# A longer warm-up of TensorE ahead of x, in float32r, with its moving data read in eight orders

## The chip, the cores and the metric

The kernel runs on one NeuronCore of a Trainium2 chip. The metric is the device time of one execution in microseconds (us), lower is better. The profile is that of one execution; its span runs from the first to the last instruction.

## The reference

`x` has the shape (2, 3008, 256). It goes through the real part of a two-dimensional Fourier transform and then, as 6,016 tokens of 256 features, through two feed-forward layers:

```python
X = np.fft.fft(np.fft.fft(x, axis=1), axis=2).real           # (2, 3008, 256)
rms = np.sqrt(np.mean(x * x, axis=-1, keepdims=True) + 1e-06) # x is now X as (6016, 256)
xn = x / rms * rms_g
g, val = xn @ w_gate, xn @ w_val                              # 256 x 1536 each
x = (g * (1 / (1 + np.exp(-g))) * val) @ w_out                # 1536 x 256
h = x @ w_in                                                  # 256 x 2048
out = (h * np.cos(h)) @ w_out2                                # 2048 x 256
```

## The kernel before

Each engine has a stream of its own, written out by hand, and semaphores order them. The stages that the prediction speaks of are these.

*Warm-up and loads.* SyncE issues ten loads of `x` (with the first table in front, the tile `front`), then the other tables and w1b, w1a, none of which waits for compute. VectorE clears a tile `zeros` of 128 columns (L928) and a single value of `stat` (L929). TensorE waits for `zeros_ready` and runs `warm_up(15)`: 15 float32 products of zeros by zeros, 128 columns each, into PSUM bank 7 (L465). A float32 product shows in the profile as two records.

*First transform along the sequence* (the first stage). VectorE folds each chunk of x as it lands (L934, L941, L944). TensorE multiplies the folded chunks, 24 pairs of rows in nine groups (L492, and L488/L489 where a chunk is only half folded), each product with 136 moving columns in float32. `warm_up(2)` stands ahead of the second and the third chunk. ScalarE copies each group out of one of six PSUM banks (L694) and turns a row of it (L702); for the last groups VectorE does part of this (L951, L959).

*Features and second transform.* Once all groups are out, TensorE runs, for each of 34 steps, the transform over features (L508) and along the sequence (L524, L526), and sums of squares (L548), all float32. In the same stretch ScalarE, VectorE and GpSimd split the first layer's weights in a high and a low float32r part.

*Main loop.* Six tiles of 502 pairs of tokens. Each product of the two layers is made of three float32r products (L561, L562, L563: high by high, high by low, low by high) of 502 moving columns. This begins at about 55 us and takes the rest of the span.

The SBUF address of `zeros` is that of buffers used later (`plus0`, one of the `pq` buffers). The moving operand of every product in this kernel is contiguous along its columns.

Of the kernel before, what the change touches and what calls it, by code (L numbers as in the profile page):

```python
# [6 lines left out]
F32 = mybir.dt.float32  # L7
F32R = mybir.dt.float32r
# [3 lines left out]
P = 128  # L12
# [12 lines left out]
N = PAIRS // PER_BATCH  # L25
# [52 lines left out]
def build(nc, x, w1a, w1b, small, wo1, win2, wo2, t_feat, t_seq2, t_const, out):  # L78
    ctx = ExitStack()
    with ctx:  # L80
# [5 lines left out]
        def sb(name, shape, at, dt=F32):  # L86
            return nc.alloc_sbuf_tensor_at(name, [P] + shape, dt, offset=base + at)
# [72 lines left out]
        o_pq = o_h + 4 * TA  # L160
        pq = [sb(f"pq{i}", [DIM], o_h + UVB + 1024 * i if i < 3 else o_pq + 2048) for i in range(4)]
        assert UVB + 3 * 1024 <= 4 * TA and 4 * N <= 2048
        zeros = sb("zeros", [P], o_pq)
        plus = [sb("plus0", [N], o_pq), sb("plus1", [N], o_x2 + 1024)]
        assert o_work + 4 * GCOLS <= o_x2 + 1024 and o_x2 + 1024 + 4 * N <= o_hid - UVB
        o_end = o_pq + pad(max(TB, 16 * DIM))
# [12 lines left out]
        ps = ctx.enter_context(nc.psum_tensor("ps", [P, 8, 512], F32))  # L179
# [24 lines left out]
        root_ready, zeros_ready = sem("root_ready"), sem("zeros_ready")  # L204
# [57 lines left out]
        def mean_rows(q):  # L262
            return sum(k.stop - k.start for _, k in PART_ROWS[:q + 1])
# [196 lines left out]
        @block.tensor  # L460
        def _(pe):

            def warm_up(count):
                for _ in range(count):
                    nc.tensor.matmul(ps[:, 7, 0:P], zeros[:, :], zeros[:, :], start=True, stop=True)  # L465

            pe.wait_ge(zeros_ready, 1)
            warm_up(15)
            pe.wait_ge(x_in[0], 16)
            for g, ms in enumerate(GROUPS):  # L470
                for i, m in enumerate(ms):
                    if m in CHUNK_AT:
                        if m:
                            warm_up(2 if CHUNK_AT.index(m) < 3 else 0)
                        pe.wait_ge(folded, CHUNK_AT.index(m) + 1)
                        if CHUNK_AT.index(m) == HALF_FOLDED[0]:
                            pe.wait_ge(seq1_turned, 4)
                    for c in group_order(g):
                        if i == 0 and g >= 3 and c == 0:
                            pe.wait_ge(n1_out, g - 2)  # L480
                        if i == 0 and g >= 3 and c == 1:
                            pe.wait_ge(row_turned, 2 * (g - 2))
                        if m == 0 and c:
                            pe.wait_ge(seq1_turned, 2)
                        acc = ps[:, n1_bank(g, c), i * COLS1:(i + 1) * COLS1]
                        even, odd = (x_sb[:, m * XM + r * P:m * XM + (r + 1) * P] for r in range(2))
                        if half_folded(m):
                            nc.tensor.matmul(acc, even, seq1_thirds[c], start=True, stop=False)  # L488
                            last = nc.tensor.matmul(acc, odd, seq1_thirds[2 * c],  # L489
                                                    start=False, stop=True)  # L490
                        else:
                            last = nc.tensor.matmul(acc, odd if c else even, seq1_thirds[c],  # L492
                                                    start=True, stop=True)
                        if i == len(ms) - 1:
                            last.then_inc(n1_done, 1)
# [429 lines left out]

        @block.vector
        def _(dve):
            nc.vector.memset(zeros[:, :], 0.0).then_inc(zeros_ready, 1)  # L928
            nc.vector.memset(stat[0:1, 0, 0:1], 1.0).then_inc(root_ready, 1)  # L929
            for i in range(XL):  # L930
                dve.wait_ge(x_in[i], 16)
# [394 lines left out]
```

## Time and profile before

| | us |
|---|---|
| median of 2 runs | 979.88 (978.4 to 981.35) |
| span of the profiled execution | 976.5 |
| warm-up, L465, first to last record's end | 1.07 to 7.12 |
| first stage on TensorE | 7.35 to 22.32 |
| features and second transform | 23.22 to 54.85 |
| main loop | 54.85 to the end |

PE is TensorE's matmuls and PEld its weight loads, DVE is VectorE, ACT ScalarE, POOL GpSimd and SP SyncE. L465 is line 465 of the kernel. A matmul record lasts longer than the distance to the next start, since matmuls overlap; the distance between starts is what one costs in a dense stream.

### The profile page before, as it was taken

The numbers are of one execution on the slowest core, as the hardware profiler recorded it, in microseconds if no ns is written. First come the engines' busy times: TensorE is split into PE (matmuls) and PEld (weight loads), VectorE is DVE, ScalarE is ACT, GpSimd is POOL, SyncE is SP. The second block draws the span as 40 slices with busy tenths as digits, with TensorE's granted clock in tenths as the row PEclk, the third lists the DMA queues.
The fourth block names the chain that finished last, engine by engine and source line by source line (L and its number), as shares of the span: only waits on it lengthen the run. The fifth ranks groups of instructions, "written<-read, shape, count | busy, mean of one in ns | idle before, by whom it ended". The sixth has DMA issues, their size and how long they took to land.

```text
span 976.5 us, 13031 instructions
## 1 busy us (share of the span) xinstructions
PE 970.6 (99%) x4530; PEld 808.5 (83%) x4530; DVE 741.0 (76%) x1029; ACT 638.4 (65%) x806; POOL 351.3 (36%) x291
## 2 busy tenths in 40 slices
PE   9999999999999999999999999999999999999998
PEld 8988888888888888888888888888888888888886
DVE  7988887678876768876768877767887667887665
ACT  5687687764378765368775358775348776447777
POOL 0477782047720027740007750006661004770000
PEclk9999999999999999999999999999999999999999
DMA  9888010000010001010001010001010000000001
GB/s 354 234 195 247 1 42 12 1 9 35 1 42 1 1 1 42 1 42 0 0 0 42 0 32 11 0 0 42 0 32 0 0 0 21 21 0 0 0 0 42
DMA packets 13794, 36.80 MB, mean 38 GB/s; under 512 B 2586, under 2 KB 6522, under 8 KB 13370
## 3 DMA queue, kind: packets, MB, share of 16 engines
q1 hardware_dynamic: 11690, 31.63, 9.3%
q0 software_dynamic: 2064, 4.72, 2.7%
q8 instruction: 15, 0.25, 0.1%
q14 instruction: 25, 0.20, 0.1%
HBM read 22.35 MB, written 9.26 MB: 32 GB/s over the span
## 4 chain that ended last, share of the span: by engine, by line
PE 97%; DMA 1%; SPq 0%; DVE 0%; ACT 0%; issue 0%
PE ps L561 31%; PE ps L562 31%; PE ps L563 31%; PE ps L508 2%; DMA front<-x 1%; PE ps L526 1%; PE ps L524 1%; SPq L332 0%; PE ps L548 0%; PE ps L492 0%; ACT g_sb L694 0%; DVE front L934 0%; ACT y_sb L923 0%; DVE front L944 0%; DVE front L941 0%
## 5 line engine op out<-in xcount | busy, mean ns | idle before, releaser
L561 PE MATMUL ps<-h_hi,wo_hi 128*128 128x502 f32 x672 | 261.5, 389 | 0.0
L563 PE MATMUL ps<-h_hi,wo_lo 128*128 128x502 f32 x672 | 261.4, 389 | 0.0
L562 PE MATMUL ps<-h_lo,wo_hi 128*128 128x502 f32 x672 | 261.2, 389 | 0.0
L1144 POOL TENSOR_TENSOR h_lo<-work,h_hi 128x502 fp32r<-128x502 f32 x92 | 102.0, 1117 | 371.6 <-ACT h_hi L822 369.8
L807 ACT ACTIVATE h_hi<-work 128x502 fp32r<-128x502 f32 x132 | 82.3, 626 | 176.7 <-POOL work L1233 176.7
L1131 DVE SCALAR_TENSOR_TENSOR work<-work,ps 128x1004 f32<-128x1004 f32 (+1 forms) x109 | 117.2, 1075 | 94.7 <-ACT work L912 94.3
L1117 DVE SCALAR_TENSOR_TENSOR work<-work,ps 128x1004 f32<-128x1004 f32 (+1 forms) x109 | 116.5, 1074 | 48.4 <-ACT work L898 48.4
L561 PE MATMUL ps<-x_hi,win_hi 128*128 128x502 f32 x384 | 149.9, 390 | 0.0
L562 PE MATMUL ps<-x_lo,win_hi 128*128 128x502 f32 x384 | 149.3, 389 | 0.0
L563 PE MATMUL ps<-x_hi,win_lo 128*128 128x502 f32 x384 | 149.2, 389 | 0.0
L561 PEld LDWEIGHTS ps<-h_hi,wo_hi 128*128 128x128 f32 x672 | 126.2, 188 | 26.9 <-DVE h_lo L1038 0.6
L562 PEld LDWEIGHTS ps<-h_lo,wo_hi 128*128 128x128 f32 x672 | 126.3, 188 | 26.0
L563 PEld LDWEIGHTS ps<-h_hi,wo_lo 128*128 128x128 f32 x672 | 126.3, 188 | 26.0
L1045 DVE SCALAR_TENSOR_TENSOR plus<-u,w,ps 128x502 f32<-128x502 f32 x144 | 105.9, 735 | 51.3 <-PE ps L563 50.7
L898 ACT ACTIVATE work<-ps 128x1004 f32<-128x1004 f32 (+1 forms) x109 | 98.3, 907 | 60.2 <-PE ps L563 59.4
L907 ACT ACTIVATE work<-work 128x1004 f32<-128x1004 f32 (+1 forms) x109 | 102.7, 943 | 31.3 <-DVE work L1117 30.4
L1233 POOL TENSOR_TENSOR work<-work,uv_t 128x502 f32<-128x502 f32 x72 | 99.7, 1411 | 45.0 <-DVE uv_t L1054 45.0
L1038 DVE TENSOR_TENSOR h_lo<-work,h_hi 128x502 fp32r<-128x502 f32 x172 | 114.3, 703 | 1.7 <-ACT h_hi L822 0.4
L561 PE MATMUL ps<-uv_hi,w_hi 128*128 128x502 f32 x288 | 112.6, 391 | 0.0
L562 PE MATMUL ps<-uv_lo,w_hi 128*128 128x502 f32 x288 | 112.0, 389 | 0.0
L563 PE MATMUL ps<-uv_hi,w_lo 128*128 128x502 f32 x288 | 111.9, 389 | 0.0
L822 ACT ACTIVATE h_hi<-work 128x1004 fp32r<-128x1004 f32 (+1 forms) x109 | 101.7, 938 | 14.9 <-PE ps L563 8.7
(96 smaller groups left out, 1269.2 us busy)
## 6 DMA issues: line engine op xcount, KB each, us to landing
out<-y_sb SPq DMA_DIRECT2D x10, 502.0 KB, 3.1
front<-x SPq DMA_DIRECT2D x4, 768.0 KB, 8.8
uv_t<-uv_dram SPq DMA_DIRECT2D x6, 502.0 KB, 3.6
front<-x SPq DMA_DIRECT2D x4, 512.0 KB, 8.9
w_lo<-w_f POOLq DMA_DIRECT2D x4, 512.0 KB, 7.5
wo_raw<-wo SPq DMA_DIRECT2D x1, 2048.0 KB, 10.9
win_raw<-win SPq DMA_DIRECT2D x1, 2048.0 KB, 8.0
raw_b<-w1b SPq DMA_DIRECT2D x3, 512.0 KB, 12.4
```

The lines of the kernel that those rows point to most:

```text
L561: nc.tensor.matmul(acc, w_hi, v_hi, start=start, stop=False)
L562: nc.tensor.matmul(acc, w_hi, v_lo, start=False, stop=False)
L563: return nc.tensor.matmul(acc, w_lo, v_hi, start=False, stop=stop)
L822: nc.scalar.activation(h_hi[j % 2][:, gs, 0:N], work[j % 4][:, gs, :], ACT.Copy).then_inc(hi_done, gs.stop - gs.start)
L898: nc.scalar.activation(work[j % 4][:, gs, :], ps[:, bank_pair(j) + gs.start:bank_pair(j) + gs.stop, 0:N], ACT.Copy, bias=MAGIC).then_inc(r ...
L907: nc.scalar.activation(work[j % 4][:, gs, :], work[j % 4][:, gs, :], ACT.Sin, scale=TURN / 2).then_inc(sin_done, gs.stop - gs.start)
L1038: nc.vector.tensor_tensor(h_lo[j % 2][:, g, 0:N], work[j % 4][:, g, :], h_hi[j % 2][:, g, 0:N].bitcast(F32), ALU.subtract).then_inc(hid_sp ...
L1045: nc.vector.scalar_tensor_tensor(out=plus[m][:, :], in0=u128[:, :], scalar=w128[:, m * C1 + i:m * C1 + i + 1], in1=ps[:, bank_pair(m), 0:N ...
L1117: nc.vector.scalar_tensor_tensor(out=buf, in0=buf, scalar=MAGIC, in1=pair, op0=ALU.subtract, op1=ALU.subtract).then_inc(frac_done, gs.stop ...
L1131: nc.vector.scalar_tensor_tensor(out=buf, in0=buf, scalar=1.0, in1=pair, op0=ALU.subtract, op1=ALU.mult).then_inc(cos_done, gs.stop - gs.s ...
L1144: nc.gpsimd.tensor_tensor(dst, src, hi.bitcast(F32), ALU.subtract).then_inc(s, 1)
L1233: nc.gpsimd.tensor_tensor(work[i % 3][:, g, :], work[i % 3][:, g, :], value[i % 2][:, g, :], ALU.mult).then_inc(h_done[g], 1)
```

## The change

`zeros` becomes a float32r tile of 1,536 columns, and the memset clears all of it. The 15 float32 products of 128 columns become 54 float32r products: 14 of 512 contiguous columns, 5 of 502, 5 of 512, and then five each of 512 columns with a step of two values, in turns of 2, of 4 and of 16 values from two stretches 512 values (2 KB) apart, with a step of three values, and with the same 8 values read 64 times. The two `warm_up(2)` inside the first stage keep 128 columns and become float32r.

```diff
-        zeros = sb("zeros", [P], o_pq)
+        zeros = sb("zeros", [1536], o_pq, F32R)
...
-            def warm_up(count):
+            def warm_up(count, moving=zeros[:, 0:P], width=P):
                 for _ in range(count):
-                    nc.tensor.matmul(ps[:, 7, 0:P], zeros[:, :], zeros[:, :], start=True, stop=True)
+                    nc.tensor.matmul(ps[:, 7, 0:width], zeros[:, 0:P], moving, start=True, stop=True)
+
+            def in_turns(run):
+                return zeros[:, 0:1024].rearrange("p (r k i) -> p k r i", r=2, i=run)[:, 0:256 // run]
 
             pe.wait_ge(zeros_ready, 1)
-            warm_up(15)
+            warm_up(14, zeros[:, 0:512], 512)
+            warm_up(5, zeros[:, 0:N], N)
+            warm_up(5, zeros[:, 0:512], 512)
+            warm_up(5, zeros[:, 0:1024:2], 512)
+            warm_up(5, in_turns(2), 512)
+            warm_up(5, in_turns(4), 512)
+            warm_up(5, in_turns(16), 512)
+            warm_up(5, zeros[:, 0:1536:3], 512)
+            warm_up(5, zeros[:, 0:8].rearrange("p (o i) -> p o i", o=1).broadcast_to([P, 64, 8]), 512)
             pe.wait_ge(x_in[0], 16)
...
-            nc.vector.memset(zeros[:, :], 0.0).then_inc(zeros_ready, 1)
+            nc.vector.memset(zeros[:, :].bitcast(F32), 0.0).then_inc(zeros_ready, 1)
```

## Rows read from the trace of the kernel before

**Rows 1.** The page: span and busy time of each engine.
```profile
span 976.5 us, 13031 instructions
PE 970.6 (99%) x4530; PEld 808.5 (83%) x4530; DVE 741.0 (76%) x1029; ACT 638.4 (65%) x806; POOL 351.3 (36%) x291
```

**Rows 2.** Chain of waits, 0 to 21 us: start, us, what.
```profile
0.75 0.40 SPq L332
...
4.91 14.17 DMA front<-x
...
19.10 0.70 DVE front L934
...
19.82 0.43 DVE front L941
...
20.28 0.44 DVE front L944
...
20.76 0.38 PE ps L492
```

**Rows 3.** Groups by form, 0 to 30 us: | busy us, mean ns | idle before.
```profile
L994 DVE TENSOR_SCALAR raw_b<-raw_b,gvec 128x512 f32<-128x512 f32 x2 | 1.0, 476 | 0.0
...
L928 DVE MEMSET zeros<- 128x128 f32 x1 | 0.2, 165 | 0.8 <-PEq L1318 0.8
...
L929 DVE MEMSET stat<- 1x1 f32 x1 | 0.1, 59 | 0.0
```

**Rows 4.** Timeline of VectorE and TensorE, 0 to 23.9 us: start, us, what [idle before].
```profile
0.85 0.17 DVE L928 MEMSET zeros<- 128x128 f32 x1 [0.85 <-PEq L1318]
...
5.06 0.96 DVE L934 TENSOR_TENSOR front<-front 128x768 f32<-128x768 f32 x1 [4.05 <-DMA front<-x]
...
1.07 6.05 PE L465 MATMUL ps<-zeros 128*128 128x128 f32 x30 [1.07 <-DVE zeros L928]
7.35 1.63 PE L492 MATMUL ps<-front 128*128 128x136 f32 x12 [0.23 <-DVE front L944]
...
14.71 1.09 PE L492 MATMUL ps<-front 128*128 128x136 f32 x8
15.64 0.40 PE L488 MATMUL ps<-front 128*128 128x136 f32 x2
...
20.76 1.72 PE L492 MATMUL ps<-front 128*128 128x136 f32 x12 [0.33 <-DVE front L944]
...
23.22 0.87 PE L508 MATMUL ps<-feat,g_sb 128*96 128x129 f32 x6 [0.74 <-ACT g_sb L694]
```

**Rows 5.** Warm-up records in three windows: duration ns min/median/max, first and last start.
```profile
L465 PE MATMUL ps<-zeros x18: 421/421/581, 1.1 to 4.9; 128*128 128x128 f32 x18
...
L465 PE MATMUL ps<-zeros x23: 414/421/581, 1.1 to 5.9; 128*128 128x128 f32 x23
...
L465 PE MATMUL ps<-zeros x8: 275/275/414, 5.9 to 6.8; 128*128 128x128 f32 x8
```

**Rows 6.** Timeline of ScalarE and VectorE at the first stage's end.
```profile
18.85 0.92 ACT L694 ACTIVATE g_sb<-ps 128x408 f32<-128x408 f32 x2
19.80 0.56 ACT L702 ACTIVATE g_sb<-ps 1x204 f32<-1x204 f32 x2
20.26 0.90 ACT L694 ACTIVATE g_sb<-ps 128x408 f32<-128x408 f32 x2
21.20 0.55 ACT L702 ACTIVATE g_sb<-ps 1x204 f32<-1x204 f32 x2
21.99 0.81 ACT L694 ACTIVATE g_sb<-ps 128x272 f32<-128x272 f32 x3 [0.24 <-PE ps L492]
...
21.40 0.29 DVE L944 SCALAR_TENSOR_TENSOR front<-front 128x128 f32<-128x128 f32 x1
```

**Rows 7.** Windows by stage: busy us (instructions) of each engine, clock, DMA.
```profile
7.34:22.32 14.98, 14.64 (x120) 14.19 (x120) 13.53 (x25) 10.61 (x30) 0.00 (x0) 1.00 1.03 393
...
23.20:54.85 31.65, 31.34 (x304) 29.77 (x305) 27.25 (x56) 20.43 (x39) 17.46 (x18) 1.00 0.87 243
54.85:100.00 45.15, 45.11 (x228) 36.37 (x229) 39.42 (x61) 35.73 (x50) 35.55 (x31) 1.00 0.76 205
100.00:976.50 876.50, 873.33 (x3849) 722.24 (x3848) 657.54 (x879) 568.97 (x681) 298.09 (x240) 1.00 0.04 13
```

**Rows 8.** Waits of TensorE: us in total, times, longest.
```profile
PE ps L465 <- DVE zeros L928: 1.1, 1, 1.1
PE ps L508 <- ACT g_sb L694: 0.7, 1, 0.7
PE ps L492 <- DVE front L944: 0.6, 2, 0.3
PE ps L548 <- issue: 0.3, 1, 0.3
```

**Rows 9.** Chain of waits at the end of the span: start, us, what.
```profile
970.84 0.23 PE ps L562
971.07 0.22 PE ps L563
971.29 0.23 PE ps L561
...
973.10 0.24 PE ps L563
```

## The prediction

> **What bounds the kernel now.** I read the page first, then the chain of waits in order of time, then the timeline of TensorE over the first stage, and last the table of stages. The page gives TensorE 99% of the span [rows 1], but that is an average, and the change sits in the first microseconds, so the question is what ends last there. The chain answers it [rows 2]. Up to 19.1 us it holds no matmul: it is the issue of the ten loads of x, then 14.17 us of transfer, then the last large fold on VectorE (19.10 to 20.72), and only then the matmuls at 20.76. The x transfer sets when the first stage can end. TensorE fits itself around it: the 15 old warm-ups run from 1.07 to about 7.1 while x is on its way, and the first stage follows from 7.35 to 22.32 [rows 4]. After 23.22 the chain is TensorE almost without a break: in the stage 23.20 to 54.85 it is busy for 31.34 of 31.65 us, and for 873.33 of 876.50 us from 100 on [rows 7], while its waits behind the first stage are 0.7 and 0.3 us [rows 8]. So what delays TensorE at 23 us delays the end by nearly the same, and what delays it before that counts only beyond the slack that the first stage has under the x transfer.
>
> **Part 1: the memset.** The tile grows from 128 to 1,536 values a partition. One column took 59 ns and 128 columns took 165 ns, so 0.83 ns a column [rows 3]; 1,536 columns give 0.059 + 1,535 x 0.00083 = 1.34 us. Bounds: 1.30 (the slope alone, nothing fixed, is 1.28) to 1.43 (the 512-column tensor_scalar, 0.93 ns a column [rows 3]). It starts at 0.85, ends at 2.19, and the first product follows 0.05 us behind its end as now (1.02 to 1.07 [rows 4]): 2.24. Behind the memset on VectorE are the 1x1 memset, which releases one ScalarE operation, and the first fold at 5.06, which waits for x [rows 3, 4]. Both are covered until 5.06; without that cover the price would be 1.2 us on each. The larger tile lies over buffers that are written only after products further down TensorE's own queue, so I see no new wait, and SyncE's and GpSimd's queues get nothing and are passed by nothing.
>
> **Part 2: the price of one new product.** It is float32r, 512 columns (five have 502). The main loop issues just such products: 502 columns, starts 0.226 us apart (ten gaps from 970.84 to 973.10 [rows 9]), so 0.450 ns a column and 0.230 us for 512. The old float32 product shows as two records; those of 136 columns start 0.116 us apart (8 in 0.93 us [rows 4]), so 0.232 us a product and 1.71 ns a column. A new product at the full clock costs about what an old one did, and there are 54 in place of 15.
>
> **The clock.** The page gives a granted clock of full speed in every slice, but the records of the warm-up say otherwise: durations of 421 ns for the first 18, 275 ns later, the change between 5.9 and 6.3 us [rows 5]. Up to there 23 records start within 4.85 us; less the longer first one (581 ns for 421) that is 22 gaps of 0.213 us, and behind it they are 0.11: the lower of the two levels (1.2 GHz), then the upper (2.4 GHz). TensorE had run without a gap for about 5.1 us when it rose. The new warm-ups are as dense and also zeros, so I let the clock rise 5.1 us after their start, at 7.35. At the lower level a product of 512 columns costs what the old float32 product of 128 cost there, 2 x 0.213 = 0.43 us (by the ratio of levels from the 0.230: 0.44).
>
> **Part 3: the length of the warm-up.** 5.1 / 0.43 = 12 products at the lower level, up to 7.4 us. The other 42 take 42 x 0.23 = 9.7 us. End at 17.1 us, against 7.1 before. This price takes the moving data's order as free. No matmul of this trace reads its moving data with a step or with jumps, so for the 30 products of the six other orders (step 2, turns of 2, 4 and 16, step 3, the same 8 values again and again) the bounds are: below, nothing extra, as in the contiguous row; above, the float32 rate, 3.8 times, 0.64 us more each, 19.3 us in all. I take nothing, because the values delivered per column are the same four bytes as in the nearest row, and keep both ends.
> The Trainium skill, page "SBUF — State Buffer", section "Specifications (TRN2)", speaks against taking nothing for all: lines of 16 bytes, and at least two hits in each for full bandwidth. By that rule step 2 (two float32 in each line) and the turns would be free and step 3 (1.3 in each) would pay; it gives no price, and no run here shows it yet.
>
> **Part 4: the first stage, late.** It starts at 17.1 + 0.1. It has 112 records (24 pairs of rows by two products, eight more for the four half-folded ones, two records each) at 0.116 = 13.0 us. By 21.7 us the last fold is done [rows 6], well ahead of its use, so the stalls that the stage has now (14.97 us less 13.0 less 8 warm-up records of 0.11 = 1.1 us) go: the stage is no longer bound by x but by TensorE. The four warm-ups inside it (2 + 2) are now float32r of 128 columns: between 0.058 us (by columns) and 0.22 (the float32 price); I take 0.11, 0.44 in all. End: 17.2 + 13.0 + 0.44 = 30.6, against 22.32: **8.3 us late**.
>
> **Part 5: what follows.** ScalarE takes 1.41 us to copy out and turn a group of three (18.85 to 20.26; 1.48 by the sum of its operations [rows 6]) and TensorE 1.39 to fill one. Today the stall at 20.4 us lets it catch up; without it its last copy ends about 0.5 us later behind the last product: +0.5. Against that, loads not gated by compute (the tables, w1a, w1b) land as early as before while their users come 8 us later, and the few gaps of TensorE between 23 and 100 us (0.31 + 0.04 us without a record at all, and some single longer steps) can shrink: -0.5. Both are small and cancel. All else is passed on, since TensorE is the chain. Its clock stays at the upper level: it works without a gap from 2.24 on.
>
> **The sum.** 8.3 + 0.5 - 0.5 = 8.3 us on this execution's span of 976.5: 984.8. The median of the runs shown is 979.88, 3.4 us over the span, so **988.2 us**.
>
> **Rivals.**
> - *Orders with a step cost by the stretch they pass over.* If skipped values are read as well, step 2 costs twice and step 3 three times: 5 x 0.23 + 5 x 0.46 = 3.5 us, 991.7; with a penalty on the turns too, up to about 995. For it: the read side then does no more per microsecond than in any row here. Against: nothing in the trace. By the page's rule just named only step 3 would pay, for which doubling is 1.2 us.
> - *Slower by over 2%: every order but the contiguous one falls to the float32 rate.* The place is the 30 products between about 10 and 17 us. The line at 999.5 us is 11.3 us above my sum, 0.38 us on each of the 30, so it decides from 2.6 times the contiguous price; at the full 3.8 times the time is 988.2 + 19.3 = 1007.5. For it: the trace has a fourfold rate for the other way of reading 4-byte data. Against: that comes with float32's two records per product, and these are float32r. The same side is reached if the clock doesn't rise under float32r zeros: 40 products at 0.43 in place of 0.23 put the start of the stage at 25.5, 8.4 us more, and part of the stage at the lower level adds several more.
> - *The delay is absorbed.* The stage's own slack (1.1 us, and 0.5 from the cheaper inner warm-ups) is in the sum. If later stages waited on transfers more than the records show, some 3 us more could vanish: 985. Against: TensorE's waits behind 23 us are a few tenths [rows 8].
> - *Longer warm-up as such does nothing for the rest*, since the clock is at the upper level from 6.2 us on already [rows 5]. So there is no way to a gain that I can price; faster has only a change of noise.
>
> **How the numbers follow.** Sum right as it stands (986 to 990.5, the clock's rise half a microsecond or so either way, 0.2 us a lower-level product): 0.50. Some orders dearer (990 to 995.5): 0.32. Absorbed (under 985.5): 0.09. Beyond the 2% line: 0.08. Faster: 0.01. The range from 984.5 to 995.5 leaves out the far side and little more; the likeliest case's own range is 986 to 990.5. With about 2% being what a measurement of this kernel tells from no change: faster 0.01, within 2% 0.91, slower 0.08.
>
> **What would show it.** The memset at 1.3 to 1.4 us; the first product near 2.2; twelve records of the warm-up 0.43 us apart and then 0.23; the first fold still at 5.06; the first matmul on x near 17; no wait of TensorE for a fold behind it; the first feature product near 31.5 in place of 23.22; the main loop's 0.226 us unchanged. Each order is a block of five, so its price can be read from the starts alone. Wrong would be: a block at twice its neighbours; more than 15 records at 0.43; a shift of the first feature product that isn't found again at the end of the span.

## The result

The changed kernel took 990.02 us (989.92 to 990.13, two runs) against 979.88 before: 1.0108 times, 95% interval 1.0068 to 1.0148. The prediction was 988.2 us with a range of 984.5 to 995.5: no change beyond 2%, on the slow side, and the measured time lies inside. Timed once more with many runs of the kernel before (21, median 978.52), it took 989.32 us (four runs), 1.0104 times [1.0086, 1.0122]. Both intervals leave out 1, so the kernel is slower by about 1%, which is under the 2% that the prediction calls a difference. The profiled execution has a span of 988.1 us against 976.5 [rows 1].

The page of the changed kernel, span and engines:

```profile
span 988.1 us, 13071 instructions
PE 981.2 (99%) x4550; PEld 814.2 (82%) x4550; DVE 742.0 (75%) x1029; ACT 638.0 (65%) x806; POOL 351.3 (36%) x291
```

Its chain of waits (start, us, what), from 0 to 40 us, beside [rows 2]:

```profile
1.14 1.35 DVE zeros L939
2.49 0.04 issue
2.53 17.98 PE ps L465 x54
20.52 1.39 PE ps L503 x12
...
29.77 1.17 PE ps L503 x10
...
33.85 0.61 ACT g_sb L705 x3
34.47 0.43 issue
34.90 1.53 PE ps L519 x12
```

The 14.17 us of x transfer that led the chain before are gone from it. In their place stand the memset and 54 products, and from there TensorE never waits for a fold. Its waits, beside [rows 8]:

```profile
PE ps L465 <- DVE zeros L939: 2.5, 1, 2.5
PE ps L519 <- ACT g_sb L705: 1.0, 1, 1.0
PE ps L559 <- issue: 0.3, 1, 0.3
```

The timeline of VectorE shows the memset and the first fold, beside [rows 4]:

```profile
1.14 1.34 DVE L939 MEMSET zeros<- 128x1536 f32 x1 [1.14 <-PEq L1329]
...
5.24 0.96 DVE L945 TENSOR_TENSOR front<-front 128x768 f32<-128x768 f32 x1 [2.75 <-DMA front<-x]
```

The first feature product starts at 34.90 us in place of 23.22, 11.68 later. The matmul that is last in the span is 11.67 later. Between the two, the difference to the kernel before stays within 0.04 us: what is late at 34 us is late at the end. (Some executions of before, c14, c24 and c54 are 3 to 5 us longer than the others of the same kernel, and the profile of c24 below is such a one.)

**The eight orders, as the profile shows them.** The warm-up's records of one block each, with duration in ns (min/median/max), first and last start:

```profile
L465 PE MATMUL ps<-zeros x3: 382/385/389, 8.6 to 9.0; 128*128 128x502 f32 x3
...
L465 PE MATMUL ps<-zeros x4: 387/395/397, 9.7 to 10.4; 128*128 128x512 f32 x4
...
L465 PE MATMUL ps<-zeros x5: 612/632/632, 10.6 to 12.4; 128*128 128x512 f32 x5
...
L465 PE MATMUL ps<-zeros x4: 500/502/503, 13.2 to 14.2; 128*128 128x512 f32 x4
...
L465 PE MATMUL ps<-zeros x5: 412/419/423, 14.5 to 15.5; 128*128 128x512 f32 x5
...
L465 PE MATMUL ps<-zeros x5: 402/402/403, 15.8 to 16.8; 128*128 128x512 f32 x5
...
L465 PE MATMUL ps<-zeros x4: 632/632/632, 17.4 to 18.8; 128*128 128x512 f32 x4
...
L465 PE MATMUL ps<-zeros x5: 378/380/398, 19.2 to 20.1; 128*128 128x512 f32 x5
```

They are, from the top: 502 and 512 contiguous, step 2, turns of 2, of 4, of 16, step 3, the same 8 values repeated. A record lasts 0.16 to 0.18 us longer than the distance to the next start; the third block's distance can be read from its own line, (12.4 - 10.6) / 4 = 0.45 us. From the starts in nanoseconds the distances are 0.223, 0.231, **0.451, 0.332, 0.250, 0.240, 0.453** and 0.219 us. Step 2 and step 3 cost twice their contiguous neighbours, which is what the prediction had named as a sign of being wrong.

### The profile page after: what moved, and what is told of

Its sections match the earlier page's. It is cut to its first block, busy times and chain, and to the rows that moved or that the text cites. A ratio compares the mean times of both kernels' runs of the same rounds, so it can differ in the third digit from the quotient of the medians.

```text
span 988.1 us, 13071 instructions
## 1 busy us (share of the span) xinstructions
PE 981.2 (99%) x4550; PEld 814.2 (82%) x4550; DVE 742.0 (75%) x1029; ACT 638.0 (65%) x806; POOL 351.3 (36%) x291
## 4 chain that ended last, share of the span: by engine, by line
PE 99%; ACT 0%; DVE 0%; issue 0%
PE ps L572 31%; PE ps L573 31%; PE ps L574 31%; PE ps L465 2%; PE ps L519 2%; PE ps L537 1%; PE ps L535 1%; PE ps L503 1%; PE ps L559 0%; ACT g_sb L705 0%; PE ps L499 0%; PE ps L500 0%; DVE zeros L939 0%; ACT g_sb L713 0%; ACT y_sb L934 0%
```

## The experiments

All kernels below except the last are the changed kernel with other lines of warm-up. `runs`, `far`, `reads` and `lanes` also clear 512 columns of `zeros` and a second tile of 2,048 in place of 1,536, and their first product starts at 3.61 us, behind both. "Distance" is that between the starts of neighbouring products; the first distance of a block, which still holds part of the change from the block before, is left out.

### Where the 10 to 12 us come from

`again` is the changed kernel as it is. `c54` reads every block contiguously:

```diff
-            warm_up(5, zeros[:, 0:1024:2], 512)
-            warm_up(5, in_turns(2), 512)
...
+            warm_up(35, zeros[:, 0:512], 512)
```

`c24` and `c14` keep the longer memset and run only `warm_up(24, zeros[:, 0:512], 512)` and `warm_up(14, ...)`.

> The changed kernel once more, timed beside the others. Theory: the warm-up ends near 20.4 us and the whole delay of the first feature product (11.7 us in the first profile) is found again at the end, so the time is 10 to 12 us over the kernel before. Rival (part of it is absorbed on the way): 5 to 8 us over it.

> The six blocks of other orders are read contiguously, the number of products stays at 54. Theory: the orders themselves cost 30 products less five times the sum of what each was above 0.23 us, 2.8 us; the warm-up ends at about 17.5 us, the span is 2.8 us under that of the changed kernel, and the time stays 7 to 9 us over the kernel before. Rival (the orders are free in the end because something else sets the stage): no difference to the changed kernel.

> 24 contiguous products in place of 54. Theory (the first stage has some 1.1 to 1.6 us of slack under the transfer of x, beyond it everything is passed on one to one): the warm-up ends at about 10.6 us, 3.5 us after that of the kernel before, and the time is 1.5 to 3 us over the kernel before. Rival (a late start is passed on in full): 3.5 us over it. Second rival (a late start is hidden under x altogether): no difference.

> Only the 14 contiguous products at the front, with the longer memset. Theory (slack under x): the warm-up ends at about 8.3 us, 1.2 us after that of the kernel before, TensorE waits for a fold at about 20.7 us as before, and the time is that of the kernel before within 1 us. Rival (passed on in full): 1.2 us over it, and no wait for a fold.

| kernel | first product on x | first feature product | time | against before |
|---|---|---|---|---|
| before | 7.35 | 23.22 | 978.52 | 1 |
| c14 | 8.54 | 23.18 | 978.00 | 0.9995 [0.9984, 1.0006] |
| c24 | 10.22 | 24.77 | 980.23 | 1.0017 [1.0002, 1.0031] |
| c54 | 17.40 | 31.95 | 987.29 | 1.0097 [1.0074, 1.012] |
| again | 19.52 | 34.07 | 989.32 | 1.0104 [1.0086, 1.0122] |
| the changed kernel's first profile | 20.36 | 34.90 | 990.02 | 1.0108 [1.0068, 1.0148] to 979.88 |

(Each ratio stands as it was recorded beside its interval; it is not exactly the quotient of the two medians.) The first feature product of c24 and of c54:

```profile
24.77 1.53 PE L511 MATMUL ps<-feat,g_sb 128*96 128x129 f32 x12 [0.96 <-ACT g_sb L697]
```

```profile
31.95 1.53 PE L513 MATMUL ps<-feat,g_sb 128*96 128x129 f32 x12 [0.96 <-ACT g_sb L699]
```

The change taken apart by count follows the prediction's picture. A start 1.2 us late (c14) costs nothing, and the rival that passes it on in full falls. One part of c14's expectation was missed: TensorE has no wait for a fold left at 20.7 us. The transfer of x is no longer in its chain, which goes from the memset through the products and then through ScalarE's copies out of PSUM:

```profile
1.14 1.35 DVE zeros L931
2.49 0.04 issue
2.53 6.17 PE ps L465 x14
...
18.01 1.17 PE ps L495 x10
19.19 0.02 issue
19.21 0.94 ACT g_sb L697 x2
...
22.14 0.61 ACT g_sb L697 x3
22.75 0.43 issue
23.18 1.53 PE ps L511 x12
```

So c14 stands about where the slack under x is used up. c24 starts its stage 2.87 us late and ends it 1.55 late, so 1.3 us of slack are used up; from c24 to c54 the start moves by 7.18 us and the first feature product by 7.18, one to one. The c54 profile has its last matmul 8.7 us later than before, as its first feature product is.

The orders' share is 2.95 us between the first feature products of the first profile and of c54, in both of which the clock rose at 7.8 to 7.9 us. Between `again` and c54 it is only 2.1. `again` is the same program as the first profile; there the clock rose at 6.2 us, so four products fewer ran at the lower level, and the first feature product came 0.83 us earlier. By time the medians of `again` and c54 are 2.0 us apart, but their intervals overlap widely: the traces show the orders' share, the timing alone wouldn't.

### What makes an order dear: four looks

After the first profile my theory was P: the read side hands over an aligned pair of neighbouring values every 0.88 ns, and a value without its neighbour takes a pair's place. It explains step 2 and step 3 at the same price (0.451, 0.453), and that same price at once refutes the prediction's rival mechanism, in which step 3 would cost more than step 2. P does not explain the turns. `low` puts the dear orders at the lower clock and adds other turns; `runs`, `far` and `reads` use the second tile, `big`. Each of these four, and `lanes` below, was timed in one execution (987.35, 995.14, 990.9, 989.27 and 993.49 us), so only their traces are read. Typical lines:

```diff
+            warm_up(3, zeros[:, 0:1024:2], 512)                                            # low
+            warm_up(5, in_turns(1), 512)                                                   # low
+            warm_up(5, big[:, 0:1024].rearrange("p (k i) -> p k i", i=4)[:, :, 1:3], 512)  # runs
+            warm_up(5, turns(2, 514), 512)                                                 # far
+            warm_up(5, big[:, 256:768], 512)                                               # reads
```

> Three products each with step 2, turns of 2 and step 3 stand at the front, at the lower clock; then 14 contiguous ones, then, at the upper clock, turns of 2, 1, 8, 32 and 128 values between the two stretches 512 values apart, five each. Theory P (the read side gives an aligned pair of neighbouring values at a fixed pace of about 0.88 ns, and a value that comes without its neighbour takes the place of a pair): at the lower clock, where a column takes 0.83 ns anyway, all orders take 0.43 us; turns of 1 take 0.45 at the upper clock. Rival S (skipped values are read too): step 2 and 3 cost 0.85 and 1.3 us at the lower clock. Theory J (each jump between stretches costs something of its own, 0.4 ns): turns of 8, 32 and 128 take 0.25, 0.235, 0.23 us.

Measured, at the lower clock: step 2 0.451, turns of 2 0.427, step 3 0.454 us. S, with 0.85 and 1.3, falls, and the 0.43 expected for all orders was missed for the two steps. At the upper clock: turns of 2 0.339, of 8 0.243, of 32 0.237, of 128 0.23, within 0.007 of J. But turns of 1, the values 0, 512, 1, 513 and so on, took **0.216 us**, less than contiguous reading. P had them at 0.45, and J's 0.4 ns for each of 511 jumps would put them at 0.43, so both fall.

> Blocks of five at the upper clock, all from one tile: contiguous; contiguous from an odd value on; two values of every four, starting at an even value; two of every four, starting at an odd one; four of every eight; step 4; the same 2, 4 and 8 values again and again. Theory P (aligned pairs): 0.23, 0.23, 0.22, 0.45, 0.22, 0.45, then 0.22 for the three. Rival K (a fixed price for each jump, wherever it goes, as turns of 2 took 0.33): both blocks of two of every four take 0.33, four of every eight 0.25 to 0.28, and repeated pairs 0.33. Rival L (a 16-byte line has to be hit twice): step 4 dearer than step 2 was (over 0.45), odd pairs as even ones.

Measured: contiguous 0.229; from an odd value 0.236; two of every four, even start, 0.454; odd start, 0.453; four of every eight 0.232; step 4 0.460; 2, 4 and 8 values repeated 0.219 each. P falls again (even pairs at 0.454), and K (repeated pairs and turns of 1 are free, though they jump at every second value or at every value). The third theory of this expectation, also called L there, is not the L below: its odd pairs as dear as even ones came true, its step 4 dearer than step 2 hardly (0.460).

> Turns between two stretches at different distances, five products each at the upper clock: contiguous; turns of 2 at 256, 512, 514, 768 and 1024 values; turns of 4 at 1024; turns of 1 at 1024 and at 514. Theory B (two stretches a multiple of 512 values, 2 KB, apart collide): turns of 2 take 0.33 us at 512 and 1024 and 0.22 to 0.24 at 256, 514 and 768. Rival K (each jump costs, whatever the distance): 0.33 for all five. Turns of 1: 0.45 by aligned pairs at both distances.

Measured: turns of 2 at 256 and 512 values 0.340, at 514 0.330 to 0.340, at 768 and 1024 0.328; turns of 4 at 1024 0.253; turns of 1 at 1024 and 514 0.216. B falls: the distance hardly matters. K's 0.33 comes near here, but K had fallen with `runs`. The 0.45 for turns of 1 was missed.

> Where the 0.23 us of a contiguous product against 0.218 of the same 8 values repeated come from. Blocks of five at the upper clock: contiguous from the tile that also holds the stationary values; contiguous from a tile elsewhere; from its value 256; from its value 1536; then the same 8, 32, 64, 128 and 256 values repeated to 512. Theory W (moving and stationary values share a stretch of memory): 0.23 for the first, 0.217 for the other three. Rival D (distance covered: each new stretch of some size costs): 0.23 for all contiguous ones, and the repeated ones rise from 0.218 to 0.23 with their length. Rival X (other engines and transfers disturb the reads): no order, with a spread inside each block.

Measured: all four contiguous blocks 0.227, once the first few products are past; the same 8 values 0.219, 32 0.236, 64 0.231, 128 and 256 0.227. W falls, and no stretch of memory is special. The distances are steady to 0.001 us for 17 contiguous products in a row, though VectorE folds and x lands at the same time, which speaks against X. Right behind the clock's rise or a change of order they are less steady, 0.224 to 0.236. The 0.231 of the changed kernel is such a block, and the 0.236 and 0.231 of the repeated 32 and 64 values may be. D's rise with the length is not seen. What is left of it: a read that meets new values all the time takes 0.227, one that stays on 8 values takes 0.219.

The records of turns of 1 in `low` (12.0 us) and of the lone odd pairs in `runs` (13.5 us):

```profile
L465 PE MATMUL ps<-zeros x5: 379/379/389, 12.0 to 12.9; 128*128 128x512 f32 x5
```

```profile
L466 PE MATMUL ps<-big,zeros x4: 629/630/637, 13.5 to 14.9; 128*128 128x512 f32 x4
```

### A theory that fits most of it, and what it forecasts

This is theory L, an estimate of a mechanism and not something that a trace shows directly. The values of a product are taken alternately by two lanes, one for the even and one for the odd places of the order. A lane holds one group of four neighbouring values (16 bytes) and needs about 1.76 ns to get the next. At the lower clock a contiguous product takes 0.427 us, 512 columns at 1.2 GHz, so one column a cycle; at 2.4 GHz that is 0.213 us, and each lane is asked for a value every 0.83 ns. Contiguous reading gives a lane two values of each group: 128 groups x 1.76 = 0.225 us (measured 0.227), just over the array's own 0.213. Step 2, 3, 4 and two of every four give a lane one value a group: 256 x 1.76 = 0.451 (0.451 to 0.460), and it is the same at the lower clock (0.451), where contiguous reading takes 0.427. In turns of 1 each lane walks through a stretch of its own, value by value, four to a group: the array sets the pace, 0.216. All this was formed on the blocks above. `lanes` puts it to new ones:

```diff
+            warm_up(5, big[:, 0:512].rearrange("p (k r i) -> p k i r", r=2, i=4), 512)
+            warm_up(5, big[:, 0:2048].rearrange("p (r k) -> p k r", r=2)[:, 0:512:2, :], 512)
...
+            warm_up(5, big[:, 0:502].rearrange("p (r k) -> p k r", r=2), 502)
```

> Theory L (formed on the blocks so far): the values of a product are read by two lanes, the even and the odd places of the order; each lane holds one stretch of four values and needs 1.76 ns to get another, while the array at the upper clock takes a value of each lane every 0.83 ns. Then it is not the step that costs but how many new groups of four a lane meets. Blocks of five at the upper clock: groups of eight read as 0, 4, 1, 5, 2, 6, 3, 7: 0.216 us by L, though no two neighbours are adjacent; two halves in turn of 1 with step 2, so 0, 1024, 2, 1026: 0.227 by L although step 2 alone took 0.451; with step 3: 0.34; with step 4: 0.45; 502 contiguous: 0.223 to 0.227; 502 as two halves of 251 in turn: 0.212; four stretches in turn of 1: 0.33 to 0.45, as turns of 2; stationary values with step 2: no more than contiguous, 0.227. Rival A (a pair is fast where its two values are adjacent or 512 and more apart, and slow at 2 to 4): the first block takes 0.45. Rival F (any step over 1 within a stretch costs a value's place): steps 2, 3 and 4 in turns all take 0.45.

The records of its blocks, in the order of the expectation, with duration and first and last start (the second window takes a neighbour's record in):

```profile
L466 PE MATMUL ps<-big,zeros x5: 378/379/379, 8.6 to 9.5; 128*128 128x512 f32 x5
...
L466 PE MATMUL ps<-big,zeros x6: 389/392/502, 9.7 to 10.9; 128*128 128x512 f32 x6
...
L466 PE MATMUL ps<-big,zeros x4: 512/514/514, 11.2 to 12.2; 128*128 128x512 f32 x4
...
L466 PE MATMUL ps<-big,zeros x5: 625/632/634, 12.5 to 14.3; 128*128 128x512 f32 x5
...
L466 PE MATMUL ps<-big,zeros x5: 390/393/417, 14.8 to 15.7; 128*128 128x502 f32 x5
...
L466 PE MATMUL ps<-big,zeros x5: 375/376/377, 16.0 to 16.8; 128*128 128x502 f32 x5
...
L466 PE MATMUL ps<-big,zeros x4: 436/449/451, 17.3 to 18.1; 128*128 128x512 f32 x4
...
L481 PE MATMUL ps<-big,zeros x5: 392/393/397, 18.4 to 19.3; 128*128 128x512 f32 x5
```

Distances: 0, 4, 1, 5 in groups of eight **0.216** (L 0.216, A 0.45); two halves in turn with step 2 **0.229** (0.227; F 0.45), step 3 **0.340** (0.34), step 4 **0.452** (0.45); 502 contiguous 0.230; 502 as two halves 0.213 (0.212); stationary values with step 2 0.231, no dearer than contiguous. Seven forecasts held to 0.004 us, and both rivals fall; four of the seven (0, 4, 1, 5, and the halves with steps) are ones that contiguous reading would not have given anyway. One did not: four stretches in turn took 0.28 us, not 0.33 to 0.45. There a lane goes to and fro between two groups, as in turns of 2 (0.328 to 0.340). If a lane kept one group only, both would be 0.45, if it kept two, 0.227. They lie between, and differ from each other. How a lane treats a group to which it comes back stays open. Nor does L give turns of 4, 8, 16 and 32 (0.250, 0.243, 0.240, 0.237, all 0.227 by L), the odd start (0.236) or the same 8 values repeated (0.219 for 0.227). And there is a rival that no run parts from L: a reader that takes the places two by two, keeps the groups of the last two and pays 1.76 ns where one of them is new gives the same forecasts for all these blocks. What is shown is what each order costs, and that new groups of four are what is paid for in the large differences; the two lanes are not proven.

### The same order in the main loop

The main loop's 4,032 products are contiguous reads of 502 values, 0.2277 us each: 876.50 us by 3849 records [rows 7]. By L it is not the array that sets this (502 columns at 2.4 GHz are 0.209). `halves` is the kernel before with one idea added:

```diff
             def three(acc, w_hi, w_lo, v_hi, v_lo, start, stop):
+                v_hi, v_lo = (a.rearrange("p (r k) -> p k r", r=2) for a in (v_hi, v_lo))
                 nc.tensor.matmul(acc, w_hi, v_hi, start=start, stop=False)
...
-                    out=plus[m][:, :], in0=u128[:, :], scalar=w128[:, m * C1 + i:m * C1 + i + 1],
-                    in1=ps[:, bank_pair(m), 0:N], op0=ALU.mult, op1=ALU.add).then_inc(plus_done, 1)
+                    out=by_two(plus[m][:, :]), in0=u128[:, :].rearrange("p (r k) -> p k r", r=2),
+                    scalar=w128[:, m * C1 + i:m * C1 + i + 1],
+                    in1=by_two(ps[:, bank_pair(m), 0:N]), op0=ALU.mult, op1=ALU.add).then_inc(plus_done, 1)
```

`by_two` views a row of 502 as 251 by 2. Tokens are columns, so reading them in another order only renames them. Four layers of products rename four times, and the gathering of the output's rows undoes it.

> The kernel before, with every product of the main loop reading its 502 moving columns as two halves of 251 in turn of 1. The columns of each result come out in that order, the u128 rows are read in the same order where they are added, and the rows of the output are gathered accordingly; nothing is left out. Theory (the main loop's 0.227 us a product are set by the pace at which a lane gets new groups of four, not by the array): 4032 products become up to 0.015 us cheaper each, up to 60 us, so 920 to 945 us, as far as VectorE and ScalarE (76% and 65% busy) keep up. Rival (it is the weight loads or other engines' reads that set it): 978 to 980 us.

It took **927.36 us** against 978.49, 0.947 times [0.9444, 0.9496]. Its windows, beside the last line of [rows 7], and the chain of waits at 500 us:

```profile
100.00:925.00 825.00, 820.03 (x3841) 719.86 (x3839) 656.11 (x877) 566.63 (x680) 293.43 (x239) 1.00 0.04 14
```

```profile
500.43 0.21 PE ps L564
500.64 0.21 PE ps L562
500.85 0.21 PE ps L563
501.06 0.21 PE ps L564
501.28 0.21 PE ps L562
```

825 us by 3841 records is 0.2148 us a product. The difference of 0.0129 us on 4,032 products is 52 us, and the span went from 976.5 to 925.4. Its weight loads last what they lasted (188 ns), the addition on VectorE that now reads and writes in another order too (734 ns against 735), and the other engines do the same work, so the rival that the loads or other engines' reads set the 0.227 us falls. That the order of the moving data sets it is shown by this one edit; that the reason is L's two lanes is argued only.

## Why the prediction was right, point by point

The class (no change beyond 2%), the side and the way from the start-up to the end were right by their mechanism. The likeliest case, orders that cost nothing, was not what happened: the case of dearer orders was, and the time came within 2 us of the sum partly by luck (last point but one).

- **What bounds the first stage, and that all beyond its slack is passed on.** Right, and shown: c14 costs nothing, c24 loses all but 1.3 us, from there on it is one to one. The slack was put at 1.1 us, and 0.5 for the cheaper inner warm-ups, 1.6 in all; 1.3 are found at the first feature product, and ScalarE's tail (below) takes 0.2 of the rest.
- **Memset.** 1.34 us forecast, 1.34 measured. But its record starts 0.29 us later (1.14 against 0.85), and that goes with its size: in all profiles with 128 columns it starts at 0.85, with 512 (`runs`, `far`, `reads`, `lanes`) at 0.93, with 1,536 at 1.14. By their ends (1.01, 1.41, 2.48) a column costs 1.04 ns, not the 0.83 that the durations gave. The price should have been read from the ends. The first product starts at 2.53, not 2.24. The first fold still starts about when x is there (5.24).
- **Price of a contiguous product and the clock.** Twelve at the lower level, forecast and seen, 0.427 us apart; 0.231 at the upper one for the forecast 0.230, and 0.227 where it is steady (c54). The price is sound, the count is luck: `again`, the same program, has eight.
- **The orders at nothing: the term that was mis-sized.** Measured extra over the contiguous 0.231 on five each: step 2 1.1 us, turns of 2 0.5, of 4 0.1, of 16 0.05, step 3 1.1, repeated -0.1: 2.8 us (2.95 against c54, whose contiguous products take 0.227). The rival with dearer orders, given 3.5 us and a chance of 0.32, came true in size but not in mechanism, since step 3 costs no more than step 2. The argument for nothing ("the values delivered per column are the same four bytes") failed: the same four bytes cost twice as much when they are met in another order; by L what counts is how many groups of four each lane meets. The Trainium skill, page "SBUF — State Buffer", section "Specifications (TRN2)", has the 16-byte line and asks for two hits in each. A group of four values fits the measurements (four of every eight 0.232 us, two of every four 0.454). Two hits are not enough as the page puts it: step 2 has them and costs 0.451 us, as does two of every four. The measurement decides: neither step 2 nor turns of 2 is free, and step 3 costs what step 2 does. Read by L, it takes two hits for each of two alternating readers, and contiguous reading of 4-byte values already sits just past that limit.
- **First stage, late.** 13.44 us forecast from its start to its last product, 13.4 measured (20.36 to 33.78). ScalarE's tail: 0.5 us forecast, 0.2 measured (the gap before the first feature product grew from 0.90 to 1.12).
- **Absorbed later: 0.5 us forecast, 0.01 measured.** In the kernel before, the listed waits of TensorE and its weight loads between 23 and 100 us are for ScalarE, for VectorE or "issue"; none is for a transfer, so there was nothing that an earlier landing could shorten.
- **From span to time.** The 3.4 us added were the median of two runs (978.4 and 981.35) less the span of one profile. With 21 runs the kernel before is at 978.52, 2.0 over that span, and in the changed kernel the difference is 1.9. So the sum was 3.3 us short on the span (0.3 memset, 2.8 orders, and 0.2 because the absorption of 0.5 didn't come while ScalarE's tail was 0.3 smaller) and 1.5 us of that was hidden by this term. The likeliest case's own range (986 to 990.5) held the time by that luck; the full range held it without.
- **Rivals.** Over 2% by the float32 rate: the dearest order costs twice the contiguous one, not 2.6 times. No rise of the clock under zeros: it rose in every profile. (Its price counts 40 products at the lower level; the warm-up has 42 behind the first twelve, and 42 give the 8.4 us that stand there.) Absorption: none.

## What to carry to other kernels

Before pricing a start-up change, find what ends last in that stage: here, under a transfer, a late start was free up to 1.3 us, and beyond that it cost its full length to the end. A page that says 99% busy doesn't say that the busy engine runs at its own pace: here each float32r product of 502 columns took 0.2277 us, and 0.2148 after a mere renaming of columns, two halves read in turn, which gave back 5% of the kernel's time. So where a kernel is a stream of equal matmuls, compare their distance with columns by clock, and measure the moving operand's order in blocks of five at the start, where it costs a microsecond or two.

## What the hardware showed that was not expected

- Moving float32r data at the upper clock: contiguous 0.227 us for 512 columns, two halves in turn 0.216, steps of 2, 3 and 4 0.451 to 0.460, turns of 2 0.33 to 0.34, turns of 4 0.25. At the lower clock step 2 and 3 still cost 0.45, contiguous 0.427. Stationary data with step 2 costs nothing here.
- The Trainium skill, page "TensorE: Matmul & The Clock Gate", section "Back-to-back issue gap", gives N / 2.4 + 2.5 ns for the isolated gap at the upper clock; for 512 columns that is 215.8 ns, an estimate from its formula. The trace agrees for turns of 1 (0.216) and not for contiguous float32r (0.227).
- The clock rose between 3.2 us (`far`, 3.61 to 6.85) and 5.8 us (`c14`, 2.53 to 8.35) after the first product; TensorE had worked without a gap from that product on. With the same program and the same start it rose at 7.9 in the first profile and at 6.2 in `again`, which alone moves the first stage by 0.83 us.
- The page's row of granted clock says full speed from the start, while durations of 628 ns before and 397 after show the rise.
